# Loading w_out in four pieces, and moving the steps of the first heads: a fused attention and two-expert-layer kernel on one core

## The reference

```python
# attention: q, k, v are (2, 8, 768, 64); 6 hash bits from proj
q_bucket, k_bucket = ...            # bits of (q @ proj > 0), (k @ proj > 0)
scores = scale * (q @ k^T);  scores = where(q_bucket == k_bucket, scores, -1e9)
x = softmax(scores) @ v             # -> 1536 tokens x 512
# first expert layer ("moe"): w1, w2 512 x 1024, w3 1024 x 1024, w_out 1024 x 512
h = ((x @ w1) * (x @ w2)) @ w3
x = h @ w_out
# second ("moe2"): four experts, weights p from domain_probs
out = sum_e p[:, e] * (relu(x @ w1[e]) @ w2[e])
```

## Time and profile before

| | |
|---|---|
| three runs | 980.22, 980.49, 981.1 us |
| the profiled execution, its own time | 981.53 us |
| its span, first to last instruction | 979.7 us |
| PE busy | 972.5 us (99%) |
| DVE, ACT, POOL busy | 602.5, 454.8, 355.5 us |
| HBM traffic | 63 GB/s over the span |

### The profile page before, as it was taken

How to read it: one execution, slowest core, us unless ns; L and a number is a source line. 1 busy time by engine, 2 the same in 40 slices (tenths; PEclk the granted TensorE clock), 3 DMA queues, 4 the chain that set the end, 5 groups by cost and what they waited for, 6 DMA issues and landing times.

```text
span 979.7 us, 15635 instructions
## 1 busy us (share of the span) xinstructions
PE 972.5 (99%) x5357; PEld 903.7 (92%) x5357; DVE 602.5 (61%) x961; ACT 454.8 (46%) x844; POOL 355.5 (36%) x348
## 2 busy tenths in 40 slices
PE   8999999999999999999999999999999999999998
PEld 6789999999999999999998988989889899898997
DVE  4769999999987780678654453443624535254342
ACT  4358888888875552554541331413405134042230
POOL 1113664656663320335171340512505216043130
PEclk9999999999999999999999999999999999999999
DMA  7536877765445330301110201102010010100102
GB/s 222 138 92 157 211 210 204 209 167 135 113 146 160 113 113 1 110 3 44 44 45 0 66 22 43 34 11 66 23 43 25 18 59 26 43 23 21 43 21 109
DMA packets 95058, 81.63 MB, mean 83 GB/s; under 512 B 33952, under 2 KB 78368, under 8 KB 95008
## 3 DMA queue, kind: packets, MB, share of 16 engines
q1 hardware_dynamic: 95008, 80.98, 29.8%
HBM read 54.69 MB, written 7.39 MB: 63 GB/s over the span
## 4 chain that ended last, share of the span: by engine, by line
PE 98%; DVE 1%; DMA 1%; issue 0%; ACT 0%; SPq 0%; DVEq 0%
PE ps L338 25%; PE ps L340 25%; PE ps L339 24%; PE ps L1580 6%; PE ps L1567 4%; PE ps L1595 3%; PE ps L1597 3%; PE ps L1569 3%; PE ps L1546 1%; PE ps L1528 1%; PE ps L1534 1%; DMA stage<-in_moe_w_out 1%; PE ps L1537 1%; DVE expo L1139 0%; DVE pT_lo L1153 0%
## 5 line engine op out<-in xcount | busy, mean ns | idle before, releaser
L736 POOL TENSOR_TENSOR v_sum<-kept,kept 128x384 f32<-128x384 f32 x48 | 49.1, 1022 | 353.7 <-ACT kept L897 353.7
L897 ACT COPY kept<-ps 128x384 f32<-128x384 f32 x144 | 68.5, 479 | 212.3 <-PE ps L340 211.4
L1441 DVE SCALAR_TENSOR_TENSOR acc<-ps,gate,acc 128x512 f32<-128x512 f32 (+1 forms) x97 | 72.2, 745 | 139.3 <-PE ps L340 139.3
L340 PE MATMUL ps<-v_hi,hid_lo 128*128 128x512 f32 (+1 forms) x388 | 150.3, 387 | 0.0
L339 PE MATMUL ps<-v_lo,hid_hi 128*128 128x512 f32 (+1 forms) x388 | 150.2, 387 | 0.0
L338 PE MATMUL ps<-v_hi,hid_hi 128*128 128x512 f32 (+1 forms) x388 | 150.1, 387 | 0.0
L1289 DVE TENSOR_TENSOR u_sum<-ps,kept 128x384 f32<-128x384 f32 x48 | 26.8, 558 | 122.6 <-PE ps L340 122.5
L1139 DVE TENSOR_SCALAR_CACHE_REDUCE expo<-ps 128x768 f32<-128x768 f32 x96 | 91.7, 956 | 13.8 <-PE ps L1569 10.4
L828 ACT ACTIVATE expo<-expo,neg_max 128x768 f32<-128x768 f32 x96 | 90.5, 943 | 7.9 <-DVE expo L1139 5.7
L1153 DVE TENSOR_TENSOR pT_lo<-ps,pT_hi 128x768 fp32r<-128x768 f32 x96 | 90.5, 948 | 3.6 <-ACT pT_hi L842 3.2
L842 ACT CAST pT_hi<-ps 128x768 fp32r<-128x768 f32 x96 | 76.6, 798 | 24.9 <-PE ps L1580 24.6
(11 more groups left out here) (169 smaller groups left out, 2377.9 us busy)
## 6 DMA issues: line engine op xcount, KB each, us to landing
w_raw<-gate_sums SPq DMA_DIRECT2D x16, 512.0 KB, 3.6
e_raw<-in_moe_w SPq DMA_DIRECT2D x64, 128.0 KB, 2.3
v_raw<-in_moe_w SPq DMA_DIRECT2D x32, 256.0 KB, 3.4
w_raw<-in_moe_w SPq DMA_DIRECT2D x48, 128.0 KB, 3.5
made_raw<-in_moe_w SPq DMA_DIRECT2D x16, 256.0 KB, 3.7
gate_sums<-made SPq DMA_DIRECT2D x8, 512.0 KB, 2.8
raw_qk<-in_q SPq DMA_DIRECT2D x16, 192.0 KB, 3.1
raw_qk<-in_k SPq DMA_DIRECT2D x16, 192.0 KB, 3.5
```

Source lines behind the costliest of these rows:

```text
L340: return nc.tensor.matmul(out_ps, lhs_lo, rhs_hi, start=False, stop=stop, skip_group_check=onto)
L736: nc.gpsimd.tensor_tensor(v_sum[:, :], kept[s][1][:, :], kept[s][2][:, :], ALU.add).then_inc(v_done, 1)
L897: nc.scalar.copy(kept[s][n][:, :], ps[4 * s + n][:, 0:HALF]).then_inc(kept_done, 1)
L1441: nc.vector.scalar_tensor_tensor(acc[:, t, cols], down_bank(h, t, n)[:, cols], gate_f[:, bass.ds(t * E + e, 1)], acc[:, t, cols], ALU.mult ...
```

## The change

Five things. The eight loads of w_out become four of two neighbouring tiles (the rows of a partition for both tiles lie side by side in memory, 4 KB instead of 2 KB), and the first two of them stand between and behind the first halves of w3. The second set of products with zeros has five instead of two. On PE the first product of tile 0 moves ahead of the transposes of tile 1's first half. On ACT and DVE the splits of w_out go in pairs, and those of tiles 4 and 5 move behind the splits of w3's second halves. In the loop over tiles 2 to 7 the steps of the first heads move within the tile: on PE step 2it-2 stands behind three products instead of ahead of them and step 2it-1 behind six; on ACT the first of the two copies moves behind the split of w3; on DVE `turn_w3(3)` moves behind `wp_low(0)`, and the codes behind the splits.

```diff
-            wout_tiles = moe_w_out.rearrange("(h p k) n -> h k p n", h=2, p=P)
+            wout_pairs = moe_w_out.rearrange("(h p j a) n -> h j p (a n)", h=2, p=P, a=2)
@@ sync
-            for it in range(2):
-                load_first_w3(it, 0)
-            for kt in range(4):
-                load_wout(kt)
+            for n in range(2):
+                load_first_w3(n, 0)
+                load_wout(n)
             for it in range(2):
                 load_first_w3(it, 1)
-            for kt in range(4, FK):
-                load_wout(kt)
+            for n in range(2, 4):
+                load_wout(n)
@@ scalar (vector alike, with w3T_low and wout_low)
             w3T_high(0, 0, first)
             wout_high(0)
+            wout_high(1)
             w3T_high(1, 1, first)
-            for j in range(1, 5):
-                wout_high(j)
-            w3T_high(0, 0, second)
-            wout_high(5)
-            w3T_high(1, 1, second)
-            wout_high(6)
-            wout_high(7)
+            wout_high(2)
+            wout_high(3)
+            w3T_high(0, 0, second)
+            wout_high(4)
+            w3T_high(1, 1, second)
+            for j in range(5, FK):
+                wout_high(j)
@@ vector
-            turn_w3(3, 1)
             for half in halves(2):
                 w3T_low(2, 0, half)
             wp_low(0)
-            for it in range(2, FK):
-                first_code(2 * it - 2)
+            turn_w3(3, 1)
+            for it in range(2, FK - 1):
                 wp_low(it - 1)
...
@@ tensor
-            run_on_zeros(2)
+            run_on_zeros(5)
+            begin_wp(0, 0)
             transpose_w3(1, first)
-            begin_wp(0, 0)
+            multiply_wp(0, 0, (1,))
             begin_wp(1, 1)
...
             for it in range(2, FK):
-                first_prep(2 * it - 2)
                 if it < FK - 1:
+                    second = 6 if it < FK - 2 else 3
                     multiply_wp(it, it % 2, range(3))
+                    first_prep(2 * it - 2)
+                    multiply_wp(it, it % 2, range(3, second))
                     first_prep(2 * it - 1)
-                    multiply_wp(it, it % 2, range(3, FK))
+                    multiply_wp(it, it % 2, range(second, FK))
```

More of the change, by code:

```diff
@@ L133, in build_program @@
         assert hid_at[0] <= cursor[0]
-        stage = [place(f"stage{n}", [P, D], F32, fold_at) for n in range(FK)]
+        stage = place("stage", [P, FK, D], F32, fold_at)
         code_f = place("code_f", [P, 2, P], F32, fold_at)
@@ L247, in build_program @@
         const_loaded, probs_loaded = sem("const_loaded"), sem("probs_loaded")
-        stage_loaded = [sem(f"stage_loaded{n}") for n in range(FK)]
+        stage_loaded = [sem(f"stage_loaded{n}") for n in range(FK // 2)]
         first_w3_loaded = [[sem(f"first_w3_loaded{n}_{h}") for h in range(2)] for n in range(2)]
@@ L345, in _, with load_wout @@
         def _(sp):
-            def load_wout(kt):
-                sp.dma_start(stage[kt][:, :], wout_tiles[kt // 4, kt % 4, :, :]).then_inc(stage_loaded[kt], 16)
+            def load_wout(n):
+                sp.dma_start(stage[:, 2 * n:2 * n + 2, :].rearrange("p a n -> p (a n)"), wout_pairs[n // 2, n % 2, :, :])\
+                    .then_inc(stage_loaded[n], 16)
             def load_first_w3(it, h):
@@ L816, in wout_high @@
             def wout_high(j):
-                act.wait_ge(stage_loaded[j], 16)
-                nc.scalar.copy(wout_hi[:, j * D:(j + 1) * D], stage[j][:, :]).then_inc(piece_hi, 1)
+                act.wait_ge(stage_loaded[j // 2], 16)
+                nc.scalar.copy(wout_hi[:, j * D:(j + 1) * D], stage[:, j, :]).then_inc(piece_hi, 1)
             def prep_copy(m, s, j):
@@ L923, in _ @@
             for it in range(2, FK):
-                first_copy(2 * it - 2)
                 wp_high(it - 1)
@@ L927, in _ @@
                     w3T_high(it + 1, (it + 1) % 2)
+                first_copy(2 * it - 2)
                 first_copy(2 * it - 1)
@@ L1120, in wout_low @@
                 dve.wait_ge(piece_hi, j + 1)
-                nc.vector.tensor_tensor(wout_lo[:, cols], stage[j][:, :], wout_hi[:, cols].bitcast(F32),
+                nc.vector.tensor_tensor(wout_lo[:, cols], stage[:, j, :], wout_hi[:, cols].bitcast(F32),
                                         ALU.subtract).then_inc(wout_split, 1)
@@ L1245, in _ @@
             wout_low(0)
+            wout_low(1)
             w3T_low(1, 1, first)
-            for j in range(1, 5):
-                wout_low(j)
[L1249 to L1253, removed]
-            turn_w3(3, 1)
+            wout_low(2)
+            wout_low(3)
+            w3T_low(0, 0, second)
+            wout_low(4)
+            w3T_low(1, 1, second)
+            for j in range(5, FK):
+                wout_low(j)
             for half in halves(2):
@@ L1257, in _ @@
             wp_low(0)
-            for it in range(2, FK):
-                first_code(2 * it - 2)
+            turn_w3(3, 1)
+            for it in range(2, FK - 1):
                 wp_low(it - 1)
[L1261 to L1264, removed]
+                w3T_low(it + 1, (it + 1) % 2)
                 if it == 2:
@@ L1268, in _ @@
                     mixing_weights()
-                first_code(2 * it - 1)
+                first_code(2 * it - 2)
                 if it + 2 < FK:
                     turn_w3(it + 2, it % 2)
+                first_code(2 * it - 1)
+            first_code(2 * FK - 4)
+            wp_low(FK - 2)
+            scale_scores(0, 0)
+            first_code(2 * FK - 3)
             scale_scores(1, 1)
@@ L1481, in multiply_wp @@
             def multiply_wp(it, par, tiles=range(FK)):
+                if not tiles:
+                    return
                 if tiles[0] == 0:
@@ L1701, in _ @@
             transpose_w3(0, first)
-            run_on_zeros(2)
+            run_on_zeros(5)
+            begin_wp(0, 0)
             transpose_w3(1, first)
-            begin_wp(0, 0)
+            multiply_wp(0, 0, (1,))
             begin_wp(1, 1)
-            for kt in (1, 2):
-                multiply_wp(0, 0, (kt,))
-                multiply_wp(1, 1, (kt,))
+            multiply_wp(1, 1, (1,))
+            for it in range(2):
+                multiply_wp(it, it, (2,))
             transpose_w3(0, second)
```

## The result

| | before | changed |
|---|---|---|
| median of 22 runs each, in turns | 980.5 us (978.41 to 982.39) | 982.12 us (981.68 to 983.96) |
| ratio, with its 95% interval | | 1.0019 (1.0012 to 1.0025) |
| profiled execution, span | 981.53, 979.7 us | 982.88, 981.1 us |
| first score matmul of head 0 starts at | 57.46 us | 58.76 us |

The changed kernel is 1.6 us slower in the medians, by the ratio 1.9 us. The forecast was 981.9 us, +1.4. Everything happens before the first score: from there to the end of the span it is 922.2 us before and 922.3 after. So the two profiles can be compared by the start of one matmul, and 1.30 us are to be explained there.

A forecast was written before the change was run, and what follows sets the result against it. PE, busy for 972.5 of 979.7 us, was taken as the bound. Terms +0.48 + 0.37 + 1.06 - 0.18 + 0.27 - 0.56 = +1.44 us on 980.49 gave 981.9 us, range 978.9 to 983.1.

The forecast's parts named there:

- start, to the transposes of tile 0's second half: Tile 1's transposes, now behind the first product, leave 2.1 fewer matmuls done before the clock rises: +0.48 us.
- piece 4: PE waits for the split of w_out's tile 4, which takes the old place of tile 5's: +0.37 us.
- piece 5: PE waits for the split of w_out's tile 5, three matmuls after tile 4's, in tile 6's old place: +1.06 us.
- projection: PE's 0.56 us wait for proj_lo at head 0's projection goes, as DVE is no longer held by POOL: -0.56 us.
- bits of head 0: Ready at U + 11.0, wanted at U + 11.1 (U: end of wp_lo of tile 0); no stall counted, no slack.
- 7.20 for it too: First w_out load lands at 7.20 us as before, since again 768 KB must be through the queue.
- the rise still at 14.2: PE's clock goes from 1.2 to 2.4 GHz at 14.2 us, as in the profile of the kernel before.
- Rival A: Clock rise needs 6.2 us of products, transposes not counting, so comes 2.2 us later: +2.5, 983.0 us, slower; chance 0.17.
- Rival B: First w_out pair lands at 5 to 5.8, products start at 6.1, rise at 7.4: -1.8, 978.7 us; chance 0.19.
- Rival C: Clock rise comes some 3.4 us earlier by itself, 1.6 us less: about 980.3 us, the same; chance 0.12.
- DVE goes first, by 0.4 us, and the 1.3 us of standing still go: DVE's w3T_lo of tile 3 starts at U + 3.2, ahead of POOL's split of head 0 at U + 3.6.
- Rival D: POOL goes first, its clash with w3T_lo stays and the bits are late: up to +0.7, 982.5 us; chance 0.08.

The follow-up runs named there:

- after_again: The changed kernel itself, unedited, measured and profiled once more: 982.39 us, ratio 1.0004 to the kernel before.
- splits: Changed kernel with the splits of w_out's tiles 4 and 5 back at their old places: 981.18 us, ratio 1.0001 to the kernel before.
- single: The kernel of both, with w_out in eight single loads at the pairs' places, same bytes in the same order: 979.98 us, ratio 0.9986.
- start_only: Kernel before with only the new start (loads, zeros, PE order, splits of tiles 0 to 3 in pairs): 979.2 us, ratio 0.998.
- before_zeros5: Kernel before with five products with zeros instead of two, nothing else changed: 980.49 us, ratio 0.999.
- before_again: The kernel before, unedited, profiled once more: 982.06 us in that profile.
- zeros2: Changed kernel with two products with zeros instead of five: 982.47 us, ratio 1.0012 to the kernel before.
- turn: Changed kernel with DVE's turn_w3(3) back ahead of the first splits of tile 2: 980.22 us, ratio 0.9992 to the kernel before.
- both: Changed kernel with the splits of w_out's tiles 4 and 5 and turn_w3(3) back at their old places: 979.29 us, ratio 0.998.

## Why the prediction was right, and where it was wrong

The time was right: 981.9 forecast, 982.12 measured. That is luck. Two of its terms were wrong, by -2.06 and +1.75 us, and cancelled each other.

| term | forecast | profile |
|---|---|---|
| start, to the transposes of tile 0's second half | +0.48 | -1.58 (15.05 to 13.47) |
| piece 4 | +0.37 | +0.38 |
| piece 5 | +1.06 | +1.07 |
| old stop of 0.18 | -0.18 | -0.18 |
| tile 2's first product | +0.27 | +0.28 (stop 0.35 to 0.63) |
| the transposes done later | 0 | +0.05 (0.25 to some 0.3) |
| projection | -0.56 | -0.48 (stop 0.72 to 0.24) |
| bits of head 0 | 0 | +1.75 |
| sum | +1.44 | +1.29 (first score: +1.30) |

**The pieces, tile 2.** Right, to 0.02 us. They were worked out as a distance from PE's own transposes, and in after_again, where PE ran at full speed from the first product on, the waits are the same; splits shows the order as their cause.

**The start: the step "7.20 for it too", and "the rise still at 14.2".** Both failed. The pair landed at 6.13. I had counted the bytes ahead, and in single they do order the landings, but took everything else as without effect, and at equal bytes single and the pair differ by 0.9 us in one profile each; rows and moment of issue are not told apart. The rise was taken from one execution as a fixed time; over all profiles it lies anywhere from ahead of the first product to 6.2 us behind it, also for one and the same code. Between medians the start is worth -2.2 us (start_only), not +0.48. I had written of the hole of 1.8 us "what fills it is only other stuff, and I cost it at nothing"; with the kernel before, filling it alone brought 1 us (before_zeros5). Two things go with it. With five or seven zeros 7 of 10 profiles had full speed from the first product on, with two 1 of 4. And a granted clock of 0.998, which in before_again was a fall in the hole, stands in 48 of 89 executions of the kernel before and in 3 of 11 with five zeros. That makes the hole the likely cause, but it is a tendency and not proof: zeros2, with a hole of 1.5 to 2.1 us, has such a fall in none of 11 and is only 0.1 to 0.4 us longer.

**Rival A** fell: in the changed kernel the rise came 3.5 us behind the first product with tile 1's four transposes in between, and in after_again it was there before them. The rule of the Trainium skill ("TensorE: Matmul & The Clock Gate", Part 4), that transposes do not count as matmuls do, did no harm that could be seen here; whether it holds, these runs don't tell. **Rival B** was half right: early data and a first product before 7, as the prediction's own mark for being wrong had it (6.92). Its time was missed, since products began at 6.92 and not at 6.1, the rise came at about 10.4 and not at 7.4, and the bits' wait came on top. **Rival C**, a rise 3.4 us earlier, is what the changed kernel's own profile has (about 10.4 instead of 14.2), together with the early data.

**The bits: the step "DVE goes first, by 0.4 us, and the 1.3 us of standing still go".** DVE did go first, but I looked at one DVE instruction alone. Behind it stood nine small ones of `constants`, and these stand still behind POOL as well. The page of the Trainium skill that the prediction named for subtractions ("SBUF — State Buffer", "Who interferes with whom") says of copies and casts, too, that they can take the shared pair if their operands meet its conditions; the trace agrees (0.92 and 2.37 us), and I had not carried it over to the instructions next in the queue. proj_lo was there at 32.96, not at U + 6.0 = 24.69 + 6.0 = 30.7; PE's projection was just served (its wait went, 0.24 of stop left), and the 2.3 us came out where the prediction had said "no slack", at the bits: at U + 13.2 instead of U + 11.0. Rival D had the place and the direction but priced the other order. The place of the bits behind tile 4's split was in the forecast; had they stayed right behind the turn, there would have been more slack for the 2.3 us (argued, not run). With the turn back in its place (turn) the wait is 0.2 and the time 1.9 to 2.2 us less, a little more than the 1.75.

**In all**, by medians: start -2.2, pieces +0.9 to +1.2, bits +1.9 to +2.2: +0.6 to +1.2, where +1.6 and +1.0 were measured. The moved steps at tile 2 and the projection are not in this sum; the terms of the table make them -0.15 us together.

## What to carry to other kernels

Where an instruction is moved out of a clash with another engine, ask what stands behind it in its queue and whether that is now in the clash; a small instruction can stand still as long as a large one. A wait that is worked out as a difference of two short chains from a common start was forecast to 0.02 us here; a term that hangs on when a load lands or the clock rises needs more than one profile of the kernel before. And a total that fits proves no term: the two wrong ones here were each larger than the effect.

## What the runs showed of the hardware

- **When TensorE's clock rises at the start of a program differs between executions of the same kernel.** Read from products of 512 columns, 0.43 us apart at 1.2 GHz and 0.23 at 2.4 GHz: the changed kernel with two products with zeros rose at about 13.1 in one profile and before 6.83 in the next; the changed kernel at about 10.4 and before 6.86; the kernel before at 14.2, and in the other profile it had risen, fell in a hole of 2.04 us and rose again at 10.7.
- **The column of the granted clock does not show the slow stretch ahead of a first rise.** It reads 1.00 there in before, after, both, single and zeros2, in windows of 1 us. A fall behind a rise does show: 0.50 from 7.5 to 10.5 us in before_again, and 0.998 as the mean of that execution.
- **Small DVE copies stand still behind POOL.** Not only the subtraction with two large inputs: four copies of 64 x 6 values took 2.37 instead of 0.75 us, a copy of 128 x 256 0.92 instead of 0.28, four subtractions of 64 x 6 values 3.03 instead of 0.74. It goes the other way too: POOL's copy q_main took 1.48 us with DVE's w3T_lo and copies beside it, and 0.83 before. In each case the DVE group ended within 0.5 us behind the POOL instruction that it ran beside.
- **The first loads.** With 768 KB through the queue at the start of the program, one load with rows of 4 KB, issued at 1.20, landed at 5.82 to 6.59 us in ten profiles; with rows of 2 KB, the last load issued at 1.67, the same bytes were in at 6.68 to 7.20 in four. Which of the two differences does it is not shown.
